# Normalised domain probabilities moved behind the first units' steps on VectorE in a fused attention and expert kernel

## The reference

```python
scores = scale * q @ k.T                       # per head, 576 x 576
thresh = max(scores, -1) - tau
scores = where(scores >= thresh, scores, -1e9)
attn = exp(scores - max(scores, -1))
attn = attn / (sum(attn, -1) + 1e-9)
x = (attn @ v)                                 # joined over heads: 2304 x 512
p = domain_probs / (domain_probs.sum(-1) + 1e-9)   # 2304 x 4
for e in range(4):
    out += p[:, e:e+1] * (relu(x @ w1[e]) @ w2[e])
```

## Time and profile before

| what | value |
|---|---|
| median of three runs | 1142.32 us (1141.06 to 1142.98) |
| the profiled execution's own time | 1141.22 us |
| its span, first to last instruction | 1139.5 us |
| TensorE busy (matmul) | 1086.4 us, 95% |
| GpSimd busy | 652.0 us, 57% |
| VectorE busy | 637.0 us, 56% |
| ScalarE busy | 585.6 us, 51% |
| HBM read and written | 102.27 MB and 4.72 MB, 94 GB/s over the span |

### The profile page before, as it was taken

How to read it: one execution, slowest core, us unless ns; L and a number is a source line. 1 busy time by engine, 2 the same in 40 slices (tenths; PEclk the granted TensorE clock), 3 DMA queues, 4 the chain that set the end, 5 groups by cost and what they waited for, 6 DMA issues and landing times.

```text
span 1139.5 us, 18609 instructions
## 1 busy us (share of the span) xinstructions
PE 1086.4 (95%) x6460; PEld 997.0 (87%) x6460; DVE 637.0 (56%) x1320; ACT 585.6 (51%) x1213; POOL 652.0 (57%) x820
## 2 busy tenths in 40 slices
PE   3767999999989999999999999999999999999998
PEld 3556998989889898998998989989899898989897
DVE  6988777778767474673755546747556321212121
ACT  5767766667676374572745735627446141414140
POOL 5967867676798275572856835718456142425250
PEclk9878999999999999999999999999999999999999
DMA  5522443443455142240424523314213132323131
GB/s 134 148 59 73 130 119 107 134 123 111 130 146 160 29 118 82 64 135 27 115 85 128 167 69 104 89 38 120 83 38 93 56 102 57 93 56 95 54 84 47
DMA packets 96284, 108.22 MB, mean 95 GB/s; under 512 B 47808, under 2 KB 51904, under 8 KB 96192
## 3 DMA queue, kind: packets, MB, share of 16 engines
q1 hardware_dynamic: 95888, 106.70, 32.8%
q10 hardware_dynamic: 304, 0.33, 0.1%
HBM read 102.27 MB, written 4.72 MB: 94 GB/s over the span
## 4 chain that ended last, share of the span: by engine, by line
PE 79%; DVE 6%; POOL 5%; DMA 4%; issue 2%; ACT 2%; SPq 1%; ACTq 0%; DVEq 0%
PE e_ps L773 11%; PE e_ps L771 11%; PE e_ps L772 11%; PE e_ps L757 10%; PE e_ps L759 10%; PE e_ps L758 10%; PE t_ps L719 6%; PE x_ps L730 3%; PE s_ps L709 3%; PE x_ps L732 3%; PE s_ps L710 3%; POOL w_lo L687 2%; DMA k_raw<-kT 2%; DVE q_hl L873 2%; DVE p L894 1%
## 5 line engine op out<-in xcount | busy, mean ns | idle before, releaser
L687 POOL TENSOR_TENSOR w_lo<-stage,w_hi 128x512 fp32r<-128x512 f32 x240 | 314.0, 1311 | 189.8 <-ACT w_hi L851 186.7
L757 PE MATMUL e_ps<-x_hi,w_hi 128*128 128x320 f32 (+1 forms) x896 | 286.0, 319 | 0.9 <-DVE h_lo L926 0.9
L759 PE MATMUL e_ps<-x_hi,w_lo 128*128 128x320 f32 (+1 forms) x896 | 280.9, 313 | 0.0
L758 PE MATMUL e_ps<-x_lo,w_hi 128*128 128x320 f32 (+1 forms) x896 | 280.7, 313 | 0.0
L771 PE MATMUL e_ps<-w_hi,h_hi 128*128 128x512 f32 x576 | 228.3, 396 | 0.0
L851 ACT ACTIVATE w_hi<-stage 128x512 fp32r<-128x512 f32 x256 | 158.0, 625 | 133.2 <-PE e_ps L773 94.1
L773 PE MATMUL e_ps<-w_hi,h_lo 128*128 128x512 f32 x576 | 225.4, 391 | 0.0
L772 PE MATMUL e_ps<-w_lo,h_hi 128*128 128x512 f32 x576 | 224.6, 390 | 0.0
L926 DVE SCALAR_TENSOR_TENSOR h_lo<-e_ps,h_hi 128x320 fp32r<-128x320 f32 (+1 forms) x224 | 111.7, 499 | 119.1 <-ACT h_hi L841 117.1
L757 PEld LDWEIGHTS e_ps<-x_hi,w_hi 128*128 128x128 f32 x896 | 168.8, 188 | 1.8 <-DVE h_lo L926 1.6
L758 PEld LDWEIGHTS e_ps<-x_lo,w_hi 128*128 128x128 f32 x896 | 169.0, 189 | 0.2
(11 more groups left out here) (56 smaller groups left out, 1534.2 us busy)
## 6 DMA issues: line engine op xcount, KB each, us to landing
stage<-w SPq DMA_DIRECT2D x256, 256.0 KB, 2.8
k_raw<-kT SPq DMA_DIRECT2D x110, 144.0 KB, 2.8
v_raw<-v SPq DMA_DIRECT2D x56, 128.0 KB, 2.2
out<-acc SPq DMA_DIRECT2D x18, 256.0 KB, 2.0
q_raw<-qT SPq DMA_DIRECT2D x16, 144.0 KB, 2.9
q_raw<-qT SPq DMA_DIRECT2D x16, 128.0 KB, 2.8
v_raw<-v SPq DMA_DIRECT2D x112, 16.0 KB, 2.2
q_raw<-qT SPq DMA_DIRECT2D x16, 112.0 KB, 2.6
```

The costliest lines, as they stand in the source:

```text
L687: gp.tensor_tensor(w_lo[:, m % RING, :], stage[:, m % STAGES, :], w_hi[:, m % RING, :], ALU.subtract).then_inc(s_wl, 1)
L757: mm(ps[:, 0:n], w_hi[:, piece, tile], x_hi[:, k, cols], start=k == 0, stop=False)
L758: mm(ps[:, 0:n], w_hi[:, piece, tile], x_lo[:, k, cols], start=False, stop=False)
L759: op = mm(ps[:, 0:n], w_lo[:, piece, tile], x_hi[:, k, cols], start=False, stop=k == KT - 1)
```

## The change

One line of `follows()`: the step `prob` now follows the row maximum of unit 4.

```diff
@@ -338,7 +338,7 @@
         return (kind, u, halves_of(u)[-1])
 
     if name == "prob":
-        return []
+        return [("max", 4)]
     if name in ("q_load", "k_load", "v_load"):
         return [(name[0] + "_lo", x - 1)] if x else []
     if name in ("q_hi", "k_hi"):
```

## The result

The changed kernel takes 1144.09 us (median of 20 runs, 1142.21 to 1148.79), the kernel before 1140.76 us (median of 20, 1138.36 to 1143.25). The ratio is 1.0033, 95% interval 1.0023 to 1.0043: slower by 3.8 us (2.6 to 4.9; the two medians differ by 3.3), where no change to be seen was forecast. The profiled execution after had a span of 1145.2 us and was one of the slower ones; single executions of one kernel spread over 5 to 7 us, so in what follows times come from the ratios, and the traces serve to find places.

The account below looks back on a forecast made before the run. TensorE bounds the expert stage; before it, nearly full VectorE and GpSimd decide when the experts start. Terms -2.3 + 3.0 - 1.2 + 0.3 = -0.2 us gave a median of 1142.1 us, range 1139.3 to 1145.0.

Parts of the forecast that it names:

- The frame: From the first expert group on TensorE is the limit; that stage moves as a block, 1030.0 us within 1.
- the worst sum: Upper extreme of the summed terms for the whole change: -1.7 + 3.7 + 1.2 = +3.2 us.
- Part 1: First queries' low part goes first, so TensorE's first product starts earlier: -2.3 us, bounds -2.85 and -1.7.
- Part 2: `prob` in VectorE's queue at unit 2's reciprocal costs +3.0 us, bounds 1.6 and 3.7.
- The third rival: At its new place `prob` is stretched by GpSimd four times, to 5.4 us: sum +2.2 us, 1144.5 us; chance 0.08.
- Part 3: VectorE's lag up to 52.00 us is partly absorbed where the chain runs over GpSimd: -1.2 us, at most -1.4.
- Part 4: End of the stretch: TensorE takes unit 26's transposes ahead of the first expert group: +0.3 us, bounds 0 and +1.2.
- The second rival: TensorE waits at unit 26's transposes before the first expert group, lag unabsorbed: +2.9 us, 1145.2 us; chance 0.12.
- The first rival: Head start stays whole, `prob` fits into VectorE's free time: -2.1 us, or -2.65 for 1139.7 us; chance 0.22.
- The fourth: TensorE's first product is held by something else, starting at 10 us or later: +1.0 us, 1143.3 us; chance 0.04.

Follow-up runs that it names:

- the split version: Old orders, not re-planned; `prob` cut in three and put into VectorE's waits in the ramp, against the kernel before: 1138.45 us, ratio 0.9984.
- the three profiles above: Old orders without `prob` (0.9985), old orders with `prob` among the experts (0.9999), that place planned anew (1.0047), each against the kernel before; same orders to unit 28.

## Why the prediction was wrong, step by step

**The frame held roughly.** After had 1032.7 us in the expert stage against 1030.0, outside the 1 us that I allowed, but kernels with the old orders had up to 1032.1 as well, so 1 us was too narrow, and the difference is near what executions vary by. (In reading I also passed over two slices at 8 tenths, the twelfth and the last; nothing hangs on it.)

**That the number fell into the range is luck.** 1144.09 us lies within 1139.3 to 1145.0. The range stood on the 1142.32 us of three runs, and over twenty the kernel before has 1140.76, 1.6 us less. As a change, +3.8 us lies above the worst sum that I had, +3.2 us.

**Part 1 was right in mechanism and place.** Forecast 8.67 us for the first product, measured 8.51. Of the lead, 2.6 us at unit 2's reciprocal, 1.7 us arrive in the time (the run without `prob`, interval 0.7 to 2.6), where I had 2.3. ScalarE did wait for the weight piece that it takes in front of the threshold of unit 2, 1.0 us up to 15.02 us, and the reciprocal of unit 2 came 2.6 us earlier all the same.

**Part 2 was right.** Forecast +3.0 on VectorE, measured 2.73. The third rival fell with it: of the four L884 (170/404/1234 ns min/median/max) two were short, one was stretched to 0.64 us behind GpSimd's normalising and one to 1.23 us behind its weight piece.

**Part 3 was right as a sum.** I had +3.0 - 1.2 = +1.8 us for `prob` at its new place; the old orders with and without it differ by 0.17%, 1.9 us. Parts 1 to 3 made -0.5 us, and the run that consists of just these measured +0.2 (-0.8 to +1.3).

**Part 4 is the step that failed.** It read: the steps of units 21 to 26 that moved stand "against" the wait at the end, bounds 0 and +1.2, taken at +0.3. I had seen in the order that steps of units 3 to 26 moved on every engine, and priced the two places that I could follow, as if the rest would even out. The moved orders were the whole loss: 0.31%, 3.5 us, with `prob` as in the change, 0.50 and 0.61% with it out or in front. The right term was a new one, "all orders of the stretch planned anew". Its sign doesn't follow from a row of before; that it could be of some us is my reading of the earlier trace rows, where VectorE and GpSimd are at 95 and 92% up to 52 us. The sum of the extremes needed it, and did not have it.

**The second rival** named the right side and one of the right places, and gave 1145.2 us. Its mechanism is not what decided: the wait in front of unit 26's transposes was 0.42 us, and taking the old end back returned some 1.4 us of 3.8, an amount that the intervals leave open. **The first rival** fell: the whole head start is worth 1.7 us, and `prob` behind unit 2 takes it back. **The fourth** fell by the first product at 8.51 us.

Which feature of the new orders costs stays open. The first product with v in front of units 6 and 7's scores is visible, and so are others; but halves and ends put back didn't add up, and one step put right on GpSimd left the kernel as slow as the change.

## What to carry to other kernels

Where one list schedule orders all engines, a small edit to one step's needs is an edit to every engine's order, and is to be priced (and tried) as such: build once with the new step placed by hand in the old orders, and once planned anew. Here three plans of three were worse than the one before; three are too few to say that any new plan is. Don't mix engines' orders from two plans: two mixtures of two cost 23 us and more. A short side computation cost nothing that could be measured in pieces, each in a wait of the engine that runs it; the ramp had such waits though the stretch behind it was full.

## What the runs showed of the hardware

A small VectorE instruction has no one price. L879, on 18 elements, took 1.27 us beside GpSimd's k step, 0.93 among the experts, 0.46 in the split version and 0.18 in the change. In the first three it ended 0.03 to 0.04 us behind the GpSimd step then in flight (8.03 against 7.99 us, 126.44 against 126.41, 8.80 against 8.76), and in the change GpSimd's step of 0.34 us ran beside it and didn't stretch it. The four L884 took 1.98 us at one place and 0.26 and 0.29 us for two each at others. The reciprocal L881 took 0.27 us every time. By the Trainium skill, "GPSIMD Engine Reference", section "8. Key points", two SBUF inputs or a 2-port mode are what contends with GpSimd. The durations agree for L884, which has two such inputs, and for L881, which has one; that L879, with one, is in a 2-port mode is shown by no run here. Where it was stretched, the price was set by what GpSimd had in hand, not by the size of the instruction.

The first queries' low part, with two inputs, is another case: 1.29 us beside GpSimd's k step, 0.42 us past that step's end, and 0.62 us alone.

TensorE's granted clock in the units' stretch was not a property of the kernel: from 24 to 52 us it was 0.88 in the profile before and 0.74 in the one with the old orders and `prob` moved, and their times are equal within 0.1%. With the same orders it was 0.91, 0.82 and 0.78 from 24 us to the experts in the three profiles above. So a late unit in one trace, with products at 0.32 us in place of 0.17, says little about the median.
